# Linear attention's scores in 64-key tiles: the upper triangle's corner left out, and the first loads reordered

## The reference

```python
gamma = 1.0 - 2.0 ** (-5.0 - np.arange(H))
for t in range(S):
    state = gamma * state + einsum('bhd,bhe->bhde', k[:, :, t], v[:, :, t])
    y[:, :, t] = scale * einsum('bhd,bhde->bhe', q[:, :, t], state)
x = y.transpose(0, 2, 1, 3).reshape(B * S, H * D)          # 3072 x 512
h = maximum(x @ w_in, 0.0); x = (h * h) @ w_out            # 2048 wide
xn = x / sqrt(mean(x * x) + 1e-6) * rms_g
out = (silu(xn @ w_gate) * (xn @ w_val)) @ w_out2          # 1536 wide
```

## Time and profile before

| | |
|---|---|
| median of three executions | 1073.17 us (1071.54 to 1074.25) |
| the profiled execution | 1073.17 us, its span 1071.3 us |
| PE busy | 1060.3 us, 99% of the span |
| DVE busy | 877.1 us, 82% |
| ACT, POOL busy | 610.0 us, 57%; 331.0 us, 31% |
| DMA | 195.76 MB, mean 183 GB/s |

### The profile page before, as it was taken

The page is one execution under the profiler, slowest core; times in us unless marked ns, Lnnn a source line. Parts: engine busy times, 40 slices in busy tenths (PEclk is TensorE's granted clock), DMA queues, the critical chain, the costliest instruction groups (busy, mean ns, idle before and its releaser), DMA issues.

```text
span 1071.3 us, 15656 instructions
## 1 busy us (share of the span) xinstructions
PE 1060.3 (99%) x5972; PEld 888.4 (83%) x5972; DVE 877.1 (82%) x940; ACT 610.0 (57%) x887; POOL 331.0 (31%) x242
## 2 busy tenths in 40 slices
PE   8999999999999999999999999999999999999998
PEld 7887888888888888888888888888888888888898
DVE  4796899878879878889889998977886986978684
ACT  2765676466765567664674545646445555444353
POOL 2753641004450005530025554005444102544000
PEclk9999999999999999999999999999999999999999
DMA  9999568763447644455652235632225761130455
GB/s 364 329 407 414 203 225 286 234 216 118 161 172 230 212 169 158 157 230 190 213 174 100 102 134 209 207 135 76 63 65 144 270 193 57 46 112 20 141 189 182
DMA packets 80697, 195.76 MB, mean 183 GB/s; under 512 B 24296, under 2 KB 34664, under 8 KB 75760
## 3 DMA queue, kind: packets, MB, share of 16 engines
q1 hardware_dynamic: 78160, 190.03, 51.2%
q10 hardware_dynamic: 2464, 4.74, 1.2%
HBM read 152.17 MB, written 42.48 MB: 182 GB/s over the span
## 4 chain that ended last, share of the span: by engine, by line
PE 94%; DMA 4%; DVE 1%; ACT 1%; issue 0%; SPq 0%; POOL 0%; ACTq 0%
PE Y L844 13%; PE Y L845 13%; PE Y L846 13%; PE Z L844 9%; PE Z L846 9%; PE Z L845 9%; PE X L844 8%; PE X L845 8%; PE X L846 8%; DMA item_scratch<-ops 2%; DMA qk_sb<-qkv 1%; PE Z L797 1%; DMA kv_sb<-qkv 1%; PE Y L771 1%; PE X L771 1%; PE Z L791 0%
## 5 line engine op out<-in xcount | busy, mean ns | idle before, releaser
L696 POOL TENSOR_TENSOR w_ops<-raw_w,w_ops 128x512 fp32r<-128x512 f32 x90 | 127.6, 1417 | 491.6 <-ACT w_ops L962 491.5
L1022 ACT CAST ops<-hid 128x1024 fp32r<-128x1024 f32 x147 | 154.7, 1053 | 162.9 <-PE Z L846 55.1
L1407 DVE TENSOR_TENSOR ops<-hid,ops 128x1024 fp32r<-128x1024 f32 x147 | 180.1, 1227 | 45.5 <-ACT ops L1022 45.0
L696 POOL TENSOR_TENSOR w_ops<-sums_w,w_ops 128x512 fp32r<-128x512 f32 x120 | 167.3, 1397 | 126.2 <-ACT w_ops L962 125.8
L844 PE MATMUL Y<-ops,w_ops 128*128 128x512 f32 x360 | 140.2, 389 | 1.3 <-ACT u L1049 1.3
L845 PE MATMUL Y<-ops,w_ops 128*128 128x512 f32 x360 | 140.1, 389 | 0.0
L846 PE MATMUL Y<-ops,w_ops 128*128 128x512 f32 x360 | 140.1, 389 | 0.0
L1058 ACT ACTIVATE gt<-gt 128x512 f32<-128x512 f32 x72 | 45.1, 632 | 111.7 <-DVE gt L1624 39.1
L844 PE MATMUL Y<-ops 128*128 128x512 f32 (+1 forms) x288 | 104.4, 362 | 0.0
L845 PE MATMUL Y<-ops 128*128 128x512 f32 (+1 forms) x288 | 104.4, 362 | 0.0
L846 PE MATMUL Y<-ops 128*128 128x512 f32 (+1 forms) x288 | 104.4, 362 | 0.0
(11 more groups left out here) (171 smaller groups left out, 2322.9 us busy)
## 6 DMA issues: line engine op xcount, KB each, us to landing
ops<-item_scratch SPq DMA_DIRECT2D x147, 512.0 KB, 4.2
raw_w<-w_f SPq DMA_DIRECT2D x30, 1024.0 KB, 5.0
item_scratch<-hid SPq DMA_DIRECT2D x30, 512.0 KB, 3.2
qk_sb<-qkv SPq DMA_DIRECT2D x23, 512.0 KB, 9.1
kv_sb<-qkv SPq DMA_DIRECT2D x20, 512.0 KB, 10.3
y_scratch<-hid SPq DMA_DIRECT2D x12, 512.0 KB, 5.9
raw<-y_scratch SPq DMA_DIRECT2D x3, 2048.0 KB, 10.4
raw<-w_b SPq DMA_DIRECT2D x5, 1024.0 KB, 5.0
```

Source lines behind the costliest of these rows:

```text
L696: nc.gpsimd.tensor_tensor(w_ops[:, k, 1], front_w_source(m, k), f32(w_ops[:, k, 0]), ALU.subtract).then_inc(w_lo, 1)
L1022: nc.scalar.copy(hop_at(n)[:, 0], hid[:, 2 * g:2 * g + 2, OPERAND[k], :]).then_inc(hop_hi, 1)
L1407: nc.vector.tensor_tensor(hop[:, 1], hid[:, 2 * g:2 * g + 2, OPERAND[k], :], f32(hop[:, 0]), ALU.subtract).then_inc(hop_lo, 1)
```

## The change

`scores(n)` computes 64-key halves. For each head, the first half of the keys meets all 128 queries, and the second half only the later 64 queries: a block of 64 keys x 64 queries above the causal diagonal isn't computed any more. Eight matmuls a chunk become sixteen, eight with 128 columns streamed and eight with 64, all in tiles 64*64. For pairs of heads of odd number the two halves of the tokens change places in the partitions of K and V (done on the host), so that the four matmuls of a group use the four quarters of the array. The blocks that aren't computed any more are set to zero once, by two memsets of VectorE in `X` and `Y`, for which TensorE waits before `scores(0)`. The mask is laid out to fit: `factors` holds two causal blocks, and grows from 68 KB to 132 KB.

At the start, the three matmuls of zeros between `scores(0)` and `scores(1)` go, and the matmul that spreads the decay stands ahead of `scores(1)`. `factors`, `tables` and the queries and keys of chunk 2 are issued on ScalarE's queue instead of SyncE's, which then holds the chunks' other loads in an order of its own.

```diff
@@ the views of the tiles
-        factors_sb = masked[:, 1, 0, 0:H + P]
-        back_sb = factors_sb[:, 0:H].rearrange("p (f a) -> p f a", f=2)
-        causal_sb = factors_sb[:, H:]
+        factors_sb = masked[:, 1, 0, 0:H + 2 * P]
+        back_sb = factors_sb[:, 0:H].rearrange("p (f a b) -> p f a b", f=2, a=2)
+        causal_sb = factors_sb[:, H:].rearrange("p (b t) -> p b t", b=2)
@@ SyncE
             load_qk(0)
-            sp.dma_start(factors_sb, factors).then_inc(factors_loaded, 16)
             load_kv(0)
-            sp.dma_start(tables_sb[:], tables).then_inc(tables_loaded, 16)
-            load_qk(2)
             load_kv(1)
-            for n in range(3, QKR):
-                load_qk(n)
-                load_kv(n - 1)
-            load_kv(KVR - 1)
+            load_qk(3)
+            load_kv(2)
+            load_kv(3)
+            load_qk(4)
+            load_kv(4)
             load_raw_w(0)
@@ TensorE, scores(n)
-                for h in range(H):
-                    rows, cols = head_rows(h), slice(P * (h // 2), P * (h // 2) + P)
-                    mm = nc.tensor.matmul(scores_ps[n % 2][:, h % 2, cols], qk_sb[rows, n % QKR, KT, cols],
-                                          qk_sb[rows, n % QKR, QT, cols], start=True, stop=True)
+                for pairs, late in product(((0, 1), (2, 3)), range(2)):
+                    for p, f in product(pairs, range(2)):
+                        keys = D * ((p + late) % 2)
+                        rows, held = slice(D * f, D * f + D), slice(P * p + keys, P * p + keys + D)
+                        cols = slice(P * p + D * late, P * p + P)
+                        mm = nc.tensor.matmul(scores_ps[n % 2][keys:keys + D, f, cols], qk_sb[rows, n % QKR, KT, held],
+                                              qk_sb[rows, n % QKR, QT, cols], start=True, stop=True)
                 mm.then_inc(scores_done, 1)
@@ TensorE, start
-            def zeros(count):
-
-                for _ in range(count):
-                    nc.tensor.matmul(R[:, 0, 0:P], y_sb[:, 2, 0:P], y_sb[:, 2, 0:P], start=True, stop=True)
-
             pe.wait_ge(zeroed, 1)
-            zeros(9)
+            for _ in range(9):
+                nc.tensor.matmul(R[:, 0, 0:P], y_sb[:, 2, 0:P], y_sb[:, 2, 0:P], start=True, stop=True)
+            pe.wait_ge(scores_zeroed, 2)
             scores(0)
-            zeros(3)
-            scores(1)
             pe.wait_ge(rows_loaded, 16)
             nc.tensor.matmul(R[:, 1, :], rows_sb[:, DM:], rows_sb[:, 0:DM], start=True, stop=True)\
                 .then_inc(decay_placed, 1)
+            scores(1)
             attend(0)
@@ ScalarE
             act.dma_start(rows_sb, decay_rows).then_inc(rows_loaded, 16)
+            act.dma_start(factors_sb, factors).then_inc(factors_loaded, 16)
             act.dma_start(qk_sb[:, 1], qkv[0, 1, :, 0:2, :]).then_inc(qk_loaded[1], 16)
+            act.dma_start(tables_sb[:], tables).then_inc(tables_loaded, 16)
+            act.dma_start(qk_sb[:, 2], qkv[0, 2, :, 0:2, :]).then_inc(qk_loaded[2], 16)
@@ VectorE
             nc.vector.memset(eps[:], EPS).then_inc(consts_set, 1)
+            for ps in (X, Y):
+                nc.vector.memset(ps[:].rearrange("p f (a t) -> p (f a) t", t=P)[:, :, 0:D], 0.0).then_inc(scores_zeroed, 1)
             dve.wait_ge(factors_loaded, 16)
             for f in range(2):
-                op = nc.vector.tensor_tensor(mask_sb[:, f, :].rearrange("p (a t) -> p a t", a=PAIRS),
-                                             causal_sb.unsqueeze(1).to_broadcast([P, PAIRS, P]),
-                                             back_sb[:, f].unsqueeze(2).to_broadcast([P, PAIRS, P]), ALU.mult)
+                op = nc.vector.tensor_tensor(mask_sb[:, f, :].rearrange("p (a b t) -> p a b t", a=2, b=2),
+                                             causal_sb.unsqueeze(1).to_broadcast([P, 2, 2, P]),
+                                             back_sb[:, f].unsqueeze(3).to_broadcast([P, 2, 2, P]), ALU.mult)
@@ host: tables and the order of K and V
+    token = np.where(odd, (t + D) % P, t)
+    causal = [1.0 * (t >= np.roll(np.arange(P), D * b)[:, None]) for b in range(2)]
+    factors = np.concatenate([back.reshape(P, H)] + causal, axis=1)
+    def odd_pairs_changed(a, pair, axis):
+        a = np.moveaxis(a, pair, 0).copy()
+        a[1::2] = np.roll(a[1::2], D, axis=axis + (axis < pair))
+        return np.moveaxis(a, 0, pair).reshape(B, CH, P, DM)
```

More of the change, by code:

```diff
@@ L190, in build @@
         decay_set = sem("decay_set")
+        scores_zeroed = sem("scores_zeroed")
         factors_loaded = sem("factors_loaded")
@@ L1812, in decay_tables @@
     rows = np.concatenate(forward + [1.0 * (t // D == (h + odd) % 2)], axis=1)
-    causal = 1.0 * (t >= np.arange(P)[:, None])
-    back = (gamma[:, None] ** -t).T.reshape(P, PAIRS, 2).transpose(0, 2, 1)
+    causal = [1.0 * (t >= np.roll(np.arange(P), D * b)[:, None]) for b in range(2)]
+    back = (gamma[:, None] ** -token).T.reshape(P, PAIRS, 2).transpose(0, 2, 1)
     by_row = gamma.reshape(PAIRS, 2).repeat(D, axis=1).T
     s = by_row[:, None, :] ** (np.arange(CH)[None, :, None] * P - S // 2)
-    k = gamma[None, None, :] ** (S // 2 - P * np.arange(CH)[None, :, None] - np.arange(P)[:, None, None])
+    k = gamma[None, None, :] ** (S // 2 - P * np.arange(CH)[None, :, None] - token.T[:, None, :])
     tables = np.concatenate([k.reshape(P, CH * H), s.reshape(P, CH * PAIRS)], axis=1)
-    factors = np.concatenate([back.reshape(P, H), causal], axis=1)
+    factors = np.concatenate([back.reshape(P, H)] + causal, axis=1)
     return [np.ascontiguousarray(a.astype(np.float32)) for a in (rows, factors, tables)]
@@ L1827, in feature_major @@
     def feature_major(a):
-        return a.reshape(B, PAIRS, 2, CH, P, D).transpose(0, 3, 2, 5, 1, 4).reshape(B, CH, P, DM)
+        return a.reshape(B, PAIRS, 2, CH, P, D).transpose(0, 3, 2, 5, 1, 4)
     def token_major(a):
-        return a.reshape(B, H, CH, P, D).transpose(0, 2, 3, 1, 4).reshape(B, CH, P, DM)
+        return a.reshape(B, PAIRS, 2, CH, P, D).transpose(0, 3, 4, 1, 2, 5)
+    def odd_pairs_changed(a, pair, axis):
+        a = np.moveaxis(a, pair, 0).copy()
+        a[1::2] = np.roll(a[1::2], D, axis=axis + (axis < pair))
+        return np.moveaxis(a, 0, pair).reshape(B, CH, P, DM)
     def front_blocks(ws, runs, per_run):
@@ L1855 @@
     q, k, v = (np.asarray(a) for a in (q, k, v))
-    qkv = np.stack([feature_major(q), feature_major(k), token_major(k), token_major(v)], axis=3)
+    qkv = np.stack([feature_major(q).reshape(B, CH, P, DM), odd_pairs_changed(feature_major(k), 4, 5),
+                    odd_pairs_changed(token_major(k), 3, 2), odd_pairs_changed(token_major(v), 3, 2)], axis=3)
     decay_rows, factors, tables = decay_tables()
```

## The result

| | before | after |
|---|---|---|
| median | 1073.14 us (six executions) | 1079.68 us (six, 1077.77 to 1081.24) |
| ratio | | 1.006, 95% interval 1.0047 to 1.0074 |
| span of the profiled execution | 1071.3 us | 1076.5 us |

The account below looks back on a forecast made before the run. It took TensorE as the bound (PE busy 99%), with DMA nearly full from about 48.5 us. Savings of 0.3 + 0.5 + 1.05 + 0.4 = 2.25 us from 1073.17 gave 1070.9 us, range 1067.5 to 1074.

Parts of the forecast that it names:

- The scores: In each chunk's scores block: 0.83 us instead of 1.09, saving 0.26 us a chunk.
- the weighing of small matmuls: In scores: sixteen more matmuls a chunk, 0.40 us if taken one after another, not paid so across tiles; saving stays 0.26.
- The cost goes by instruction: Rival for scores, 5 in 100: 38 ns a matmul, 0.11 to 0.12 us more a chunk, 1075.5 us in all.
- The start: Up to chunk 5: chunk 0 ends 1 to 1.5 us earlier, hidden by the 3.05 us wait; 0.3 us counted for earlier loads.
- After the wait: From scores(5) to 48.5 us: TensorE sets the pace, saving 0.5 us at 1.2 GHz plus 1.05 us in later chunks.
- DMA decides from 48 us on: From 48.5 to 104 us: full DMA leaves 0.4 us to gain until 60 us, nothing after.
- the second rival: VectorE takes over, 15 in 100: 93% busy from 60 to 76.7 us, no room for 3.07 us chunks; 1072 us.
- The clock: Rival around the wait before scores(5), 12 in 100: clock recovers 3 us sooner, 1069.4 us, or later, 1072.4 us.

Follow-up runs that it names:

- Half the keys: New scores with only the first of each head's two matmuls, start and loads of the kernel before: 1073.5 us, ratio 0.9993 to 1.0015.
- small loads: From chunk 5 on, loads bring 32 of 512 columns, start and loads' order of before: new scores 1067.9 us, old scores 1067.8.

## Why the prediction was wrong

- **The scores: right.** The changed block takes 0.83 us and a chunk 3.08, as worked out; the four-tile rounds of 64 columns cost 0.06 us:

```profile
39.48 0.90 PE L773 MATMUL Y<-qk_sb 64*64 64x128 f32 x32
40.31 0.69 PE L820 MATMUL R<-kv_sb,k_dec 128*64 128x64 f32 x16
...
42.56 0.90 PE L773 MATMUL X<-qk_sb 64*64 64x128 f32 x32
```

- **The step that failed** is the weighing of small matmuls. From the four starts within 0.04 us I concluded that a matmul more costs nothing on the array, which is so, and then counted the 32 added instructions of a chunk at nothing altogether. I named no cover for them. The cover was the block of 256 that arrives in time: 6.7 us of work a block before, 4.9 after, where from one block's end a full DMA takes 2.6 to 5.0 us to start the packet, 1.0 to move it, and TensorE goes on 1.24 to 1.61 us later. The rival *The cost goes by instruction* had the sign, and the wrong mechanism and size: 2.3 us spread evenly, where the changed kernel has six pauses of 0.45 to 2.54 us at block ends.
- **The start: wrong inside, harmless outside.** I had chunk 0 earlier by 1 to 1.5 us. `factors` came at 7.52 instead of 5.87, the second chunk's queries at 10.10, and the load behind chunk 0 was issued at 14.52, 2.8 us later than before. Five loads of 512 KB and the larger `factors` are now issued in the first 3 us; that they delay each other is my reading, and wasn't tried apart. The wait before `scores(5)`, now 0.45 us, took it up, and with no long wait there the clock stayed at 2.4 GHz (1.00 in the second stretch above). The slow work only moved ahead: after the wait of 3.17 us at 10.10 the clock is 0.86 over 0 to 24 us, and 0.14 x 24 is 3.4 us, as much as 0.48 x 7 before. The new start alone measures 0.9986 to 1.0005.

```profile
7.52 1.29 DVE L1375 TENSOR_TENSOR mask_sb<-masked 128x512 f32<-128x512 f32 x2 [5.39 <-DMA masked<-factors]
...
10.10 1.56 PE L773 MATMUL Y<-qk_sb 64*64 64x128 f32 x32 [3.17 <-DMA qk_sb<-qkv]
...
14.52 0.33 SPq L429 DMA_DIRECT2D qk_sb<-qkv  x1
...
25.60 0.90 PE L773 MATMUL Y<-qk_sb 64*64 64x128 f32 x32 [0.45 <-DMA qk_sb<-qkv]
```

- **After the wait.** The load behind chunk 9 is issued at 45.73 us, 1.0 us earlier than before; I had 0.3 + 0.5 + 1.05 = 1.85.
- **DMA decides from 48 us on: right in what it excluded, incomplete.** Half the keys, with 0.5 us a chunk less, ended the attention only 2.0 us earlier and brought nothing at the end. With DMA's load taken away, the waits for VectorE grew, as the second rival had it, and of 4.4 us saved 1.7 were left at chunk 21; so a faster `scores` had two covers over it, and I had put only 15 in 100 on the second.
- **The clock.** After the pause of 2.54 us for instructions it is 0.50 from 80 to 84 us, and 0.87 over the whole stretch from 76.7 us, where the kernel before has 1.00.

The books: PE's waits up to 120 us are 16.2 us where they were 7.9, 8.3 more: the 8.4 us for instructions, while the others cancel. PE is busy for 1056.7 us on the page instead of 1060.3, 3.6 less, where 24 x 0.26 = 6.2 us of columns were saved; work at 1.2 GHz would account for the rest. That leaves 4.7 of the 5.2 us between the spans. Of the 8.4 us, the 3.3 before 57 us cost nothing at chunk 12; the three pauses behind it are 5.1 us.

The trace shows when a packet starts, not when it is asked for. That it starts within 1.0 us of a block's end with small loads, and 2.6 to 5.0 after it in the changed kernel, says that the full DMA is what holds it up; a request that is late by itself would be late with small loads too. What the 1.24 to 1.61 us from a landing to the next matmul consist of stays open.

## What to carry to other kernels

Count instructions as well as columns: where matmuls are small and DMA is full, 32 more fp32 instructions in 3 us cost more than the columns that they save. Pauses of PE "by issue" inside a loop without waits, 256 instructions apart or a multiple (some 250 in a count of matmuls and weight loads), are the sign. And before a stage's main engine is made faster, take away its next bound in a run (here the loads) and see whether anything moves; here about 5 us came off with the old scores, and the faster scores added nothing to it.

## What was not expected of the hardware

- TensorE's instruction supply held at 49 instructions a microsecond with DMA at a share of 0.34. At 49 to 52 with DMA mostly at 0.95 or more it failed at three to six of the seven blocks' ends from 48 to 95 us, in the four kernels of 160 instructions a chunk with full loads; in the run with fewer stores three passed in a row at 0.88 to 1.01. At 38 it held at 1.03 in the kernel before, and failed once, for 0.7 us, with the new start alone; with 64 queries left out (39) it failed once, for 0.5 us.
- Weights of 128 columns make a round of 64 streamed columns as long as one of 128 (0.11 us); weights of 64 columns on four tiles let it take 0.06.
- Four matmuls in what had been a 3 us wait kept the clock at 2.4 GHz (1.00 over 24 to 31 us instead of 0.52), and 1 us of it reached the end.
